# Attention and two MLP layers in fp32 precision: MLP tiles of 768 tokens in place of 384, with both layers' weights streamed through a ring of four chunks

## The reference

```python
scores = scale * np.matmul(q, k.transpose(0, 1, 3, 2))
scores = np.where(block_i >= block_j, scores, -1e9)
attn = softmax(scores)                       # rows, with + 1e-09 in the sum
x = np.matmul(attn, v)                       # heads beside each other: (2304, 512)
h = x @ w_in                                 # layer 1: 512 -> 2048
x = (h * (1.0 / (1.0 + np.exp(-h)))) @ w_out          # 2048 -> 512
h = x @ w_in2                                # layer 2, the same sizes
out = (h * (1.0 / (1.0 + np.exp(-1.702 * h)))) @ w_out2
```

## Time and profile before

| | |
|---|---|
| time, median of 3 runs | 1059.19 us (1058.28 to 1060.75) |
| profiled execution: span from first to last instruction | 1056.4 us |
| what lies around the span (median less span) | 2.8 us |
| TensorE (PE) busy | 1002.8 us, 95% |
| weight loads (PEld) busy | 945.6 us |
| VectorE (DVE) busy | 482.4 us, 46% |
| ScalarE (ACT) busy | 378.5 us, 36% |
| GpSimd (POOL) busy | 201.7 us, 19% |
| mean granted TensorE clock | 0.984 |
| moved by DMA | 36.22 MB |

### The profile page before, as it was taken

The page is one execution under the profiler, slowest core; times in us unless marked ns, Lnnn a source line. Parts: engine busy times, 40 slices in busy tenths (PEclk is TensorE's granted clock), DMA queues, the critical chain, the costliest instruction groups (busy, mean ns, idle before and its releaser), DMA issues.

```text
span 1056.4 us, 16256 instructions
## 1 busy us (share of the span) xinstructions
PE 1002.8 (95%) x5936; PEld 945.6 (90%) x5936; DVE 482.4 (46%) x999; ACT 378.5 (36%) x874; POOL 201.7 (19%) x133
## 2 busy tenths in 40 slices
PE   5887797799999999999999999999999999999998
PEld 4665565567999999999999999999999999999998
DVE  7978878885633333233323464323323333232322
ACT  5755565564222222222222222222222222232222
POOL 7535534521900000000000388000000000000000
PEclk9989988999999999999999999999999999999999
DMA  4222222201400000000000133000000000000000
GB/s 161 91 65 76 67 65 76 65 23 52 140 21 1 1 1 0 0 0 0 0 1 1 40 120 120 1 2 30 1 1 30 0 30 0 0 31 1 30 1 30
DMA packets 16057, 36.22 MB, mean 34 GB/s; under 512 B 1680, under 2 KB 5776, under 8 KB 16016
## 3 DMA queue, kind: packets, MB, share of 16 engines
q1 hardware_dynamic: 16016, 35.66, 10.2%
HBM read 30.93 MB, written 4.72 MB: 34 GB/s over the span
## 4 chain that ended last, share of the span: by engine, by line
PE 87%; DVE 8%; issue 3%; DVEq 0%; DMA 0%; ACT 0%
PE ps_s L464 13%; PE ps_y L480 13%; PE ps_s L465 13%; PE ps_y L479 13%; PE ps_y L481 13%; PE ps_s L466 13%; PE ps_y L415 4%; PE ps_y L431 4%; PE ps_s L395 3%; DVE p_sb L645 3%; DVE nmax L672 2%; DVE den_e L631 2%; DVE rden L636 0%; DMA q_raw<-qT 0%; DVE pt_last L625 0%
## 5 line engine op out<-in xcount | busy, mean ns | idle before, releaser
L728 DVE TENSOR_TENSOR g_lo<-g_f,g_hi 128x384 fp32r<-128x384 f32 x192 | 120.5, 628 | 282.0 <-ACT g_hi L583 282.0
L723 DVE TENSOR_TENSOR g_f<-ps_s,sig 128x384 f32<-128x384 f32 x192 | 107.0, 557 | 229.3 <-ACT sig L577 228.9
L583 ACT ACTIVATE g_hi<-g_f 128x384 fp32r<-128x384 f32 x192 | 101.0, 526 | 302.9 <-PE ps_y L481 285.4
L577 ACT ACTIVATE sig<-ps_s 128x384 f32<-128x384 f32 x192 | 94.4, 492 | 251.8 <-PE ps_s L466 251.8
L464 PE MATMUL ps_s<-x_hi,w_lo_a 128*128 128x384 f32 x384 | 128.5, 335 | 0.0
L466 PE MATMUL ps_s<-x_lo,w_hi_a 128*128 128x384 f32 x384 | 128.3, 334 | 0.0
L465 PE MATMUL ps_s<-x_hi,w_hi_a 128*128 128x384 f32 x384 | 128.3, 334 | 0.0
L481 PE MATMUL ps_y<-g_lo,w_hi_b 128*128 128x384 f32 x384 | 128.3, 334 | 0.0
L479 PE MATMUL ps_y<-g_hi,w_lo_a 128*128 128x384 f32 x384 | 128.3, 334 | 0.0
L480 PE MATMUL ps_y<-g_hi,w_hi_a 128*128 128x384 f32 x384 | 128.3, 334 | 0.0
L481 PE MATMUL ps_y<-g_lo,w_hi_a 128*128 128x384 f32 x384 | 128.3, 334 | 0.0
(11 more groups left out here) (64 smaller groups left out, 1690.5 us busy)
## 6 DMA issues: line engine op xcount, KB each, us to landing
w_raw<-w_chunks SPq DMA_DIRECT2D x32, 512.0 KB, 3.3
q_raw<-qT SPq DMA_DIRECT2D x16, 288.0 KB, 2.8
v_sb<-v_main SPq DMA_DIRECT2D x16, 256.0 KB, 2.5
yT<-x_f SPq DMA_DIRECT2D x5, 768.0 KB, 3.7
k_raw<-kT SPq DMA_DIRECT2D x8, 288.0 KB, 3.1
w_raw<-kT SPq DMA_DIRECT2D x8, 288.0 KB, 3.1
yT<-x_f SPq DMA_DIRECT2D x4, 192.0 KB, 1.9
v_sb<-v_tail SPq DMA_DIRECT2D x16, 32.0 KB, 2.4
```

What stands on the lines that cost most here:

```text
L577: nc.scalar.activation(sig[:, f % 2, :], ps_s[:, 512 * (f % 4):512 * (f % 4) + TT], ACT.Sigmoid, scale=ALPHA[m]).then_inc(s_sig, 1)
L583: nc.scalar.activation(g_hi[:, f % 2, :], g_f[:, :], ACT.Copy).then_inc(s_gh, 1)
L723: nc.vector.tensor_tensor(g_f[:, :], ps_s[:, 512 * (f % 4):512 * (f % 4) + TT], sig[:, f % 2, :], ALU.mult).then_inc(s_g, 1)
L728: nc.vector.tensor_tensor(g_lo[:, f % 2, :], g_f[:, :], g_hi[:, f % 2, :].bitcast(F32), ALU.subtract).then_inc(s_gl, 1)
```

## The change

The MLP takes tiles of 768 tokens, three per layer. Each product of 768 columns is issued as a matmul of 512 columns (`MAIN`) and one of 256 (`SIDE`). The output's main parts fill the four banks of `ps_y`, and its side parts lie in two banks of `ps_s`, two to a bank; the hidden value of 768 columns takes the other two banks of `ps_s`, once, so that `hidden` runs one chunk ahead and waits for the `gate` of the chunk before. The split weights no longer stay: `w_hi` and `w_lo` are rings of four chunks, and all 16 chunks of a layer are loaded and split anew in each of its three tiles, 96 in all. In the attention loop GpSimd splits no chunks any more; chunk 0 is split before the loop as before, chunk 1 behind its last turn. K of the odd pairs has a buffer of its own. The MLP's code is written out instead of looped.

```diff
-TT = 384
-NT = TOK // TT
+TT = 768
+MAIN = 512
+SIDE = TT - MAIN
+NT = TOK // TT
+NTILES = 2 * NT
+NCHUNK = NTILES * NF
+RING = 4
...
-        w_hi_a = sb(ctx, "w_hi_a", [P, HALF * CW], F32R)
-        w_lo_a = sb(ctx, "w_lo_a", [P, HALF * CW], F32R)
+        w_hi = sb(ctx, "w_hi", [P, RING, CW], F32R)
+        w_lo = sb(ctx, "w_lo", [P, RING, CW], F32R)
...
-        k_raw = (sb(att, "k_raw0", [P, S]), w_raw[:, 1, 0:S])
+        k_raw = (sb(att, "k_raw0", [P, S]), sb(att, "k_raw1", [P, S]))
...
-        sig = sb(ctx, "sig", [P, 2, TT])
+        sig = sb(ctx, "sig", [P, TT])
...
# SP
+            def load_chunk(c):
+                if c >= 2:
+                    sp.wait_ge(s_w, c - 1)
+                sp.dma_start(w_raw[:, c % 2, :], w_chunks[(c // (NT * NF)) * NF + c % NF, :, :]).then_inc(s_raw[c % 2], 16)
...
             with sp.Fori(3, PAIRS // 2) as it:
                 load_qk(2 * it, 0, True)
                 load_v(2 * it - 3, 1, True)
                 load_qk(2 * it + 1, 1, True)
-                load_chunk(it, 0, it)
                 load_v(2 * it - 2, 0, True)
...
+            for c in range(2, NCHUNK):
+                load_chunk(c)
+                t = c // NF - NT - 1
+                if c % NF == 6 and t >= 0:
+                    a = tokens_of(t)
+                    sp.wait_ge(s_ea, 3 * (NT + t + 1))
+                    sp.wait_ge(s_ed, 3 * (NT + t + 1))
+                    sp.dma_start(y_out[:, :, a:a + TT], x_kt[:, :, a:a + TT]).then_inc(s_out, 16)
...
# GpSimd
+            def split_chunk(c):
+                pool.wait_ge(s_raw[c % 2], 16 * (c // 2 + 1))
+                if c >= RING:
+                    pool.wait_ge(s_y, c - RING + 1)
+                nc.gpsimd.tensor_copy(w_hi[:, c % RING, :], w_raw[:, c % 2, :]).then_inc(s_whi, 1)
                 pool.wait_ge(s_whi, c + 1)
+                nc.gpsimd.tensor_tensor(w_lo[:, c % RING, :], w_raw[:, c % 2, :], w_hi[:, c % RING, :].bitcast(F32),
+                                        ALU.subtract).then_inc(s_w, 1)
             def turn(it, last=False):
                 low_parts(2 * it, 0)
                 scale_q(2 * it + 1, 1, it)
-                chunk_high(it, 0, it + 1, w_hi_a[:, at])
                 low_parts(2 * it + 1, 1)
                 if not last:
                     scale_q(2 * it + 2, 0, it + 1)
-                chunk_low(it, 0, w_hi_a[:, at], w_lo_a[:, at])
...
+            for c in range(1, NCHUNK):
+                split_chunk(c)
...
# TensorE
+            def hidden(c):
+                t, f = c // NF, c % NF
+                pe.wait_ge(s_w, c + 1)
+                if f == 0:
+                    pe.wait_ge(s_xl, NK * (t + 1))
+                if c:
+                    pe.wait_ge(s_g, c)
+                hi, lo = w_hi[:, c % RING, :], w_lo[:, c % RING, :]
+                for a, b in ((0, MAIN), (MAIN, TT)):
+                    for k in range(NK):
+                        w = slice(P * k, P * k + P)
+                        dst = ps_s[:, a:b]
+                        nc.tensor.matmul(dst, lo[:, w], x_hi[t % 2][:, k, a:b], start=(k == 0), stop=False)
+                        nc.tensor.matmul(dst, hi[:, w], x_hi[t % 2][:, k, a:b], start=False, stop=False)
+                        last = nc.tensor.matmul(dst, hi[:, w], x_lo[t % 2][:, k, a:b], start=False, stop=(k == NK - 1))
+                last.then_inc(s_h, 1)
...
+            def output(c, final=False):
+                t, f = c // NF, c % NF
+                pe.wait_ge(s_gl, c + 1)
+                if f == 0 and t:
+                    pe.wait_ge(s_ea, 3 * t)
+                    pe.wait_ge(s_ed, 3 * t)
...
+            pair(PAIRS, 0, PAIRS // 2, cur=False, also={5: first_hidden})
             pair(PAIRS + 1, 1, PAIRS // 2, cur=False, prev=False)
+            pe.wait_ge(s_xe, 2 * PAIRS)
+            for c in range(NCHUNK):
+                if c + 1 < NCHUNK:
+                    hidden(c + 1)
+                output(c, c == NCHUNK - 1)
...
# ACT; DVE has the same order with gate, g_low and its own pieces
+            def take_output(t):
+                a = tokens_of(t)
+                act.wait_ge(s_y, NF * (t + 1))
+                for k in range(2):
+                    nc.scalar.activation(x_kt[:, k, a:a + MAIN], main_bank(k), ACT.Copy).then_inc(s_ea, 1)
+                nc.scalar.activation(x_kt[:, 0:2, a + MAIN:a + TT], side_bank(0), ACT.Copy).then_inc(s_ea, 1)
...
+            for c in range(NCHUNK):
+                t, f = c // NF, c % NF
+                sigmoid(c)
+                g_high(c)
+                if f == 0 and t:
+                    take_output(t - 1)
+                if f in (4, 6, 8, 10) and t + 1 < NTILES:
+                    split_x(t + 1, f // 2 - 2)
+            take_last()
```

More of the change, by code:

```diff
@@ L356, in _ @@
             scale_q(2, 0, 1)
[L357 to L358 removed]
+            split_chunk(0)
             with pool.Fori(1, PAIRS // 2 - 1) as it:
@@ L479, in output @@
-                    nc.tensor.matmul(dst, lo[:, w], g_hi[:, f % 2, :], start=(f == 0), stop=False)
-                    nc.tensor.matmul(dst, hi[:, w], g_hi[:, f % 2, :], start=False, stop=False)
-                    last = nc.tensor.matmul(dst, hi[:, w], g_lo[:, f % 2, :], start=False, stop=(f == NF - 1))
-                    if final and f == NF - 1:
-                        last.then_inc(s_k_done, 1)
-                if not (final and f == NF - 1):
-                    last.then_inc(s_y, 1)
@@ L487, in tile @@
-            def tile(t, par, m, m_next, final):
-                for f in range(NF):
-                    if f + 2 < NF:
-                        hidden(par, m, f + 2)
-                    elif not final:
-                        if f + 2 == NF:
-                            pe.wait_ge(s_xl, NK * (t + 2))
-                        hidden(1 - par, m_next, f + 2 - NF)
-                    output(t, f, final)
-            def first_hidden(f):
+                    dst = main_bank(k)
+                    nc.tensor.matmul(dst, lo[:, w], g1[:, 0:MAIN], start=(f == 0), stop=False)
@@ L612, in _ @@
-            act.wait_ge(s_xe, H)
-            pair(PAIRS, 0, PAIRS // 2, cur=False, ahead=False, also={k: (lambda k=k: split_x(0, 0, k)) for k in range(NK)})
-            for f in range(2):
-                sigmoid(f, f, 0)
-                g_high(f, f)
-            mlp_tiles(act, tile)
+                    nc.scalar.activation(x_kt[:, k, a:a + MAIN], main_bank(k), ACT.Copy).then_inc(s_ea, 1)
+                act.wait_ge(s_k_done, NK + 1)
+                nc.scalar.activation(x_kt[:, 0:2, a + MAIN:a + TT], side_bank(0), ACT.Copy).then_inc(s_ea, 1)
@@ L620, in _ @@
+            act.wait_ge(s_xe, 2 * H)
+            pair(PAIRS, 0, PAIRS // 2, cur=False, ahead=False, also={k: (lambda k=k: split_x(0, k)) for k in range(NK)})
+            for c in range(NCHUNK):
[7 more added lines that the diff above has]
+            take_last()
         @block.vector
@@ L758, in _ @@
-            pair(PAIRS, 0, PAIRS // 2, cur=False, also={k + 1: (lambda k=k: split_x(0, 0, k)) for k in range(NK)})
+                    nc.vector.tensor_copy(x_kt[:, k, a:a + MAIN], main_bank(k)).then_inc(s_ed, 1)
+                dve.wait_ge(s_k_done, NK + 2)
+                nc.vector.tensor_copy(x_kt[:, 2:4, a + MAIN:a + TT], side_bank(1)).then_inc(s_ed, 1)
+            pair(PAIRS, 0, PAIRS // 2, cur=False, also={k + 1: (lambda k=k: split_x(0, k)) for k in range(NK)})
             def first_gate():
-                gate(0, 0)
-                g_low(0, 0)
+                gate(0)
+                g_low(0)
@@ L763, in _ @@
             pair(PAIRS + 1, 1, PAIRS // 2, cur=False, prev=False, also={3: first_gate})
             take_pv(PAIRS - 1, 1)
-            dve.wait_ge(s_xe, 2 * PAIRS)
-            dve.sem_inc(s_ed, 1)
-            gate(1, 1)
-            g_low(1, 1)
-            mlp_tiles(dve, tile)
+            for c in range(1, NCHUNK):
+                t, f = c // NF, c % NF
+                gate(c)
+                g_low(c)
+                if f == 0:
+                    take_output(t - 1)
+                if f in (4, 6, 8, 10) and t + 1 < NTILES:
+                    split_x(t + 1, f // 2 - 2)
```

225 lines of the change are left out of this document (73 added, 152 removed).

## The result

The changed kernel takes 1040.8 us (median of 4 runs, 1039.5 to 1041.7); the kernel before took 1058.7 in the same comparison (4 runs, 1058.0 to 1060.8). The ratio is 0.982, with a 95% interval from 0.980 to 0.984. Forecast were 1038.3 us and a range of 1028 to 1054.

What follows compares the result with a forecast made beforehand. It took TensorE as dense in the MLP but held in attention by DVE multiplies that wait for GpSimd's instructions. Terms -26.3 + 1.2 + 1.6 + 2.3 + 0.3 = -20.9; 1056.4 - 20.9 + 2.8 = 1038.3 us, range 1028 to 1054.

Steps and rivals of the forecast that it cites:

- The attention iterations: Attention loop without GpSimd's chunk splits: short and long iterations both become 13.42 us; -26.3 in all, bounds -18.1 and -30.9.
- The cold stretches: Attention iterations with a stretch at 1.2 GHz, 1.54 us each: 3 of 13 assumed to stay cold, +4.6.
- Chunk 1: Its split behind turn 7 makes DVE's small L631 and multiplies come later: +1.2 us, 0 to 2.4.
- The end of attention: Wider split_x, merged early hidden chunks and the wait for the last take_pv: +1.6 us together, 0.7 to 3.
- the same columns: End of attention: one early hidden chunk of 24 matmuls replaces two of 12, with columns unchanged.
- The matmul widths: MLP pairs of 512 and 256 columns against two of 384: +1 ns a pair, 2.3 us, bounds -6 and +17.
- Rival 1: MLP: the 512-column matmul is dear, +7 ns per pair in place of +1, +14 us, 1052; chance 0.17.
- rival 2: Attention loop: another instruction of the chain is late at once, eating the gain; 1065, or 1059; chance 0.06.
- rival 3: MLP: a weight load takes its recorded 188 ns, longer than a 256-column matmul; +157, about 1195; chance 0.03.
- rival 4: MLP: the weight stream makes TensorE wait in each chunk; with 0.5 us a chunk +48, 1086; chance 0.06.
- the cover set aside for that: MLP: a g_low that met GpSimd's subtract adds 2.2, 7.1 of 8.3 us, leaving cover of 1.2 us.
- The 2.8 of the sum: Time outside the profiled span or between executions: the median 1059.2 is 2.8 us above the span 1056.4.

Runs made afterwards that it cites:

- experiment 1: Changed kernel with GpSimd's cast and subtract put back into turns 1 to 7 of the attention loop, no loads added: 1071.5 us.
- experiment 2: Changed kernel with only GpSimd's cast put back into turns 1 to 7 of the attention loop: 1055.7 us.
- experiment 3: Changed kernel with only GpSimd's subtract put back into turns 1 to 7, and one cast ahead of the loop: 1061.4 us.
- experiment 4: Changed kernel with five weight loads of chunk 1 put back into SP's attention loop, no GpSimd work: 1039.4 us.
- experiment 11: Changed kernel with chunk 1 split only after DVE's last row maxima, not right behind turn 7: 1040.8 us.
- experiment 9: Changed kernel with TensorE's wait for attention's last output copy moved from hidden(1) to output(0), and g_low(0) behind the last take_pv: 1039.4 us.
- experiment 10: Changed kernel with the moved wait of experiment 9 and hidden(0) issued in two parts, 512 columns then 256 later: 1038.6 us, ratio 0.981.
- experiment 5: Kernel before, 384-column tiles and resident weights kept, with only the chunk splits and their loads moved out of the attention loop: 1032.6 us, ratio 0.975.
- experiment 6: Changed kernel with each output chunk's 256-column part issued ahead of its 512-column part, last chunk as before: 1037.6 us, ratio 0.980.
- experiment 7: Changed kernel with output alternating three matmuls of 512 columns and three of 256: 1043.1 us.
- experiment 8: Changed kernel without loads and splits of chunks 4 to 95, later chunks computing with the first four chunks' weights: 1039.4 us.

## Why the prediction was right, and where it was off

**The attention iterations** were right in mechanism and size. Forecast were iterations of 13.42 and three of 13 cold; that is what came, and the iterations sum to 174.4 us against 200.56 less 26.3, or 174.3. Experiments 1 to 4 tie it to GpSimd's two instructions: the casts give 14.2, the subtracts 17, the loads nothing. That they meet to 0.1 is partly luck: in the ten kernels here whose loop is free of these instructions (all but before and experiments 1 to 3) the 13 iterations sum to 172.8 to 174.5, and the first alone takes 10.3 to 13.0. The 1.0 us by which the row in the table differs is 0.9 at the start: the loop's first `k_hi` is at 20.17, and at 19.28 before. In the profiled executions of all fourteen kernels told of here it lies anywhere from 19.1 to 20.4, so I put that down to scatter. The lower bound of that term, 18.1, is 18.2 by its own products, which changes nothing. The Trainium skill, "SBUF — State Buffer", section "Who interferes with whom", has VectorE and GpSimd share a port pair that one instruction holds to its end, in either direction. The traces agree in both: 0.24 us became 2.34 on DVE (experiment 1), and 1.04 became 3.58 on GpSimd (experiment 11).

**The cold stretches** were only counted, not explained. The prediction's three of 13 were a guess. In the free loops here, one to three of the 12 iterations from 30 us on hold a stretch at 1.2 GHz, which costs 1.54 us, although TensorE's idle time ahead of `pt_last` is only 1.8 us in each. With the cast back (experiment 2) seven are cold. One such stretch more or less is of the size of the distance between runs of one kernel (1039.5 to 1041.7). What decides in which iteration it falls is open.

**Chunk 1** was mis-sized: +1.2 in the sum, 0.2 by experiment 11. The cast does stand there, but it holds the multiplies just ahead of `pt_last` by only 0.2 (the pair takes 0.65 us, and 0.43 in experiment 11); the subtract behind it holds an L602 (1.21 us in place of 0.15) for which TensorE doesn't wait.

**The end of attention** was mis-sized: +1.6 in the sum, with 0.7 to 3 as bounds. Less the 0.2 for chunk 1, +4.5 was measured, above the upper bound. Four waits make up most of it.

- The wider `split_x` holds `hidden(0)` up by 1.0, as forecast (0.9).
- The last copy costs 1.5 and not 0.7, since `g_low(0)` at 768 columns stands ahead of it on DVE; experiment 9 takes that away and gets 1.6 back.
- Another 1.0 was not in the sum at all: `hidden(1)` had filled a hole between the last pairs, and merging two early hiddens into one left it open. The sentence "the same columns" was true and hid it; experiment 10 fills the hole and gets 1.1 back.
- TensorE's last wait for `pt_last` is 1.43 against 0.72 before. It has nothing to do with the wide tiles: it is 1.43 in experiment 5 too, whose stretch of 39.48 from the last `k_hi` is 0.75 longer than the 38.73 of before. It is 1.22 in experiment 11, so 0.2 of it is chunk 1's cast. The other 0.5 is a hold again. Before, two of DVE's multiplies ran between GpSimd's two `q_lo`; now the two `q_lo` (from 196.89 on, 2.98 us) follow each other and hold the multiplies to their end. DVE's timelines before and after:

```profile
223.52 0.57 DVE L645 TENSOR_SCALAR p_sb<-p_sb,rden 128x256 f32<-128x256 f32 x2
```

```profile
198.25 1.74 DVE L616 TENSOR_SCALAR p_sb<-p_sb,rden 128x256 f32<-128x256 f32 x2
```

Experiments 5 and 11 have 1.73 and 1.74 there. What lets one or the other go first wasn't looked into. Some 0.5 of the 4.7 us are in no wait.

**The matmul widths** were nearly right: +2.3 forecast, +3.9 measured, 1.7 ns a pair against 1. The cadence of 226.7 and 120.0 is the equal 13.3 ns that the prediction started from. What came on top is the change of width. The 237 ns of one score group is near the 234 and 236 of the first two here, but the other group stood at 227 in the same place, so those rows didn't show it and this study doesn't settle them. Experiments 6 and 7 move it down and up (796.5, 798.4, 800.3) with the same matmuls. Rival 1 was thus true of the first matmuls of a group and of no others; at 7 ns a pair it would have cost 16.

**The rivals.** The attention gain wasn't eaten (rival 2). A weight load doesn't take its recorded 188 ns (rival 3): 256 columns with a load each follow at 120.0. The Trainium skill, "TensorE: Matmul & The Clock Gate", section "LDWEIGHTS (loading the stationary operand)", has columns divided by 1.2, an estimate of 107 ns for 128 columns; the 120.0 leaves room for that. The weight stream makes TensorE wait nowhere (rival 4): experiment 8 has the same stream without it. `g_low` takes 957 to 959 ns in all 96 chunks: no single one met a GpSimd instruction, where one of before took 2.77, and the cover set aside for that was not needed. That is the ring's doing, and the prediction hadn't seen it. GpSimd's cast waits for a free slot, so in the stream it always starts when TensorE's `output` ends (all 92 casts are released by L471), and `g_low` is over by then. Around 606 us `g_low` runs from 604.73 to 605.69, the cast starts at 606.22, and the subtract behind it ends at 609.73. How it would be if they did meet in each chunk, no run shows.

**What lies outside the span** is 1.7 to 1.8 us in the four executions of the changed kernel. The 2.8 of the sum held besides that 1.0 by which the profiled execution before was faster than the median. The profiled execution after is 1.0 slower than its median, so spans differ by 16.4 and medians by 18.0. That the time was missed by only 2.5 is therefore in part luck: which executions were profiled made up for 2 us. The error in the span is 4.5: 1.0 in attention, 1.9 behind it (chunk 1 was put 1.0 too high and the end of attention 2.9 too low), 1.6 in the matmuls.

## What to carry to other kernels

An edit that does two things should be timed in its halves. Here all of the gain, and more, lay in taking GpSimd's long instructions out of a loop in which DVE's small ones are on the path (1032.6 alone, 1040.8 with the wider tiles); such a hold shows in a trace as one form of instruction with durations ten times apart (the narrow multiply, 0.24 and 2.35 us) whose long ones end with an instruction of the other engine. Look for it again afterwards: GpSimd's own work for attention still holds DVE here (the pair of multiplies of 1.74 us above). When work that fills a hole is merged or moved, look at the trace for the hole, even if the sum of columns stays. And where a stream of matmuls has two widths, put those of one width together.

## What the runs showed of the hardware that was not expected

A change of matmul width has a price. After matmuls of 256 columns the first five of 512 take 28.1 ns more than five steady ones, after 512 the first two of 256 take 7.5 less: 21 ns for each change and back with groups of twelve, 10 with groups of three. It is paid in starts and shows as no wait.

An idle time of 1.8 us of TensorE, once in 13.4 us, was sometimes followed by a stretch at 1.2 GHz and mostly not: one to three times in 12 iterations, in ten kernels. With a longer wait (the cast) in every other iteration it was seven in 12.

DVE's subtracts, one right behind the other, held a cast of GpSimd over all three (3.58 us in place of 1.04, of which 0.9 came behind them). GpSimd got no turn between them.
